# Folded logits copied to SBUF by ScalarE and turned by VectorE later in the loop

## The chip, the cores and the metric

The kernel runs on one core of one Trainium2 chip. A core has TensorE (matmuls, reading SBUF and writing PSUM), VectorE, ScalarE and GpSimd (called POOL in the profile), a queue for DMA transfers (SyncE), the on-chip memory SBUF and the accumulator memory PSUM with its eight banks of 128 x 512 f32. The engines run side by side, each in its own written order, and meet at semaphores: one instruction raises a counter, another engine waits for a value. The metric is the device time of one execution in microseconds (us), the median of several runs.

## The reference

Three blocks in a row: an attention with a decaying state, a gated MLP, and a mixture of experts with 32 slots. The slots' logits are used twice: over all tokens (a softmax down the 3072 tokens) and within a token (a softmax over the 32 slots).

```python
def _attn_ref(r, k, v, w, u):                # 4 x 8 heads, 768 tokens, 48 wide
    for t in range(S):
        cur = np.einsum('bhd,bhe->bhde', u[None] * kt, vt)
        y[:, :, t] = np.einsum('bhd,bhde->bhe', rt, state + cur)
        state = wt[:, :, :, None] * state + np.einsum('bhd,bhe->bhde', kt, vt)

def _moe_ref(x, w_in, w_out):                # 3072 x 384, inner width 2048
    h = x @ w_in
    g = h * np.clip(h + 3.0, 0.0, 6.0) / 6.0
    return g @ w_out

def _moe2_ref(x, phi, w1, w2):               # 8 experts x 4 slots, inner width 1024
    logits = x @ phi
    d = np.exp(logits - logits.max(0, keepdims=True))
    d /= d.sum(0, keepdims=True) + 1e-09
    slot_input = d.T @ x                     # then two matmuls per expert
    c = np.exp(logits - logits.max(1, keepdims=True))
    c /= c.sum(1, keepdims=True) + 1e-09
    return c @ slot_out
```

## The kernel before

**Tiles and stages.** The 768 positions are cut into six chunks of 128 (`C` = 6), each for the four batches (`B` = 4): 24 attention units. Four units make a token group of 512 tokens. The first four units run ahead of the loop. The loop then takes 96 steps (`STEPS`), 16 (`FT`) for each of the six token groups. In step s, with `g, i = divmod(s, FT)`, TensorE computes tile i of the MLP's hidden layer for group g: nine f16 matmuls of 128 x 512 into `hid` (`mlp`, L602; a high and a low half each of weights and x stand in for f32). ScalarE takes the clipped part (`relu_step`, L1473), VectorE multiplies (`gate`, L1075) and turns the product (`turn_gated`, L1096) into a ring of tiles. The matmuls of step s wait for the gate of step s - 2. Beside that, one attention unit of a later group is worked on every four steps (`unit_of`; phases 0 to 3).

**The attention unit on the engines.** Phase 0: TensorE's `score` (L500) waits for the decayed keys and receptances of POOL; VectorE finishes the output of the unit before (`finish_y`, L1035, which waits for POOL's `diag_values`, L1663) and adds its state (L1044). Phase 1: VectorE masks the scores (L1016) and scans a prefix (L962), ScalarE makes their high half (`high_scores`, L1380), and TensorE turns x (`turn_x`, L599), for which it waits for `finish_y`. Phase 2: TensorE turns the keys (L510), ScalarE copies them to SBUF (`copy_keys`, L1394), and TensorE makes the state increment with them (`increment`, L529). Phase 3: TensorE attends (L575 to L592); VectorE scans the suffix (L975), from which POOL decays the keys of the next unit (`decay_keys`, L1678). The loop's increments and key turns end with unit 19, which is worked on in group 3.

**The logits of a group.** `w_out @ phi` is folded into `w_phi`, so the logits come straight from the gated tiles. `add_logits` (L664) adds them up in one PSUM bank, `l_ps`, four tiles at a time, in four parts of 32 rows each. The last four are added in step 0 of the next group. Then, all for group g - 1 and in group g:

- step 1: ScalarE and VectorE split `l_ps` into a high and a low half (L1486, L1104; both lie in the SBUF tile `l_part`, which is a part of `soft3`, "soft" in the profile), and TensorE sums the four parts back into `l_ps` (`fold_logits`, L695, L696), waiting for both halves;
- step 2: VectorE takes the maximum (L1110), ScalarE the exponential (`weigh`, L1497) and from the second group on the factor `alpha` (L1503), and VectorE turns the weights (`turn_weight`, L1141);
- step 2, or step 4 for the last two groups of the five: VectorE turns the logits themselves into SBUF in four 32 x 128 transposes out of `l_ps` (`turn_logits`, L1119), for the second softmax;
- step 3: TensorE gathers the slots (`gather_slots`, L727), 64 matmuls into four banks, one of which is `l_ps` for groups 0 to 2 (for groups 3 and 4 it is `inc_ps`, free by then: `idle_inc`);
- step 4: VectorE adds the slot sums (`add_slots`, L1165);
- step 5: TensorE starts on the next logits in `l_ps`.

So `l_ps` has to be empty for the gather, where that writes it, and for the next logits. TensorE waits for `logits_done` in both places. The sixth group has code of its own.

**What sets the order.** Every engine's order is written out by hand: each engine's block has its own `for s in range(END)` with conditions on the phase, on g and on i. Nothing is rearranged afterwards.

## Time and profile before

| | us |
|---|---|
| median of 3 runs | 411.77 (411.71 to 412.57) |
| profiled execution | 412.07 |
| its span, first to last instruction | 410.1 |
| TensorE busy | 391.4 (95%) |
| VectorE busy | 333.9 (81%) |
| ScalarE busy | 198.4 (48%) |
| POOL busy | 217.5 (53%) |
| mean granted clock of TensorE | 0.992 of full speed |

The loop starts at about 36 us and ends at about 357 us; expert weights and outputs take the rest. A busy share is an average: what an edit is worth is read at the place it touches, from who waits there for whom. A row of the timeline gives the start, the duration, the engine, the line, the operation with output and input, and in square brackets how long the engine had been idle and what released it. On TensorE the durations overlap, since matmuls are pipelined: a 128 x 512 matmul is listed with 0.38 us and the next starts 0.22 later. On ScalarE and VectorE neighbours overlap by up to about 0.1 us too.

### The profile page before, as it was taken

What the parts mean: (1) busy time and instruction counts of PE and PEld (TensorE: products, weight loads), DVE (VectorE), ACT (ScalarE), POOL (GpSimd) and SP (SyncE); (2) the same over time, 40 slices, a digit from 0 to 9 for tenths busy, and PEclk for the clock granted to TensorE, in tenths of its full rate; (3) what the DMA queues carried; (4) which work ended last, traced back from release to release, by engine and by line L of the source; (5) the groups of instructions that cost most, each with busy time, mean ns of one, the idle gap of its engine ahead of it and who ended that gap; (6) DMA issues with size and microseconds to landing.
All of it is one profiled execution on the core that took longest, in us unless ns stands there. A gap on an engine that the chain in (4) does not pass through costs nothing.

```text
span 410.1 us, 10077 instructions
## 1 busy us (share of the span) xinstructions
PE 391.4 (95%) x3977; PEld 210.0 (51%) x3977; DVE 333.9 (81%) x536; ACT 198.4 (48%) x408; POOL 217.5 (53%) x206
## 2 busy tenths in 40 slices
PE   7999999999999999999999999999999999999981
PEld 3885555455455554555554555554444444543430
DVE  7998799998999898998989998989876887661251
ACT  3576355545545757366554556653533234321141
POOL 2444988978468777658774687775650012010000
PEclk9999999999999999999999999999999999999996
DMA  8999412439242134124430331232007199779929
GB/s 236 336 410 315 135 32 97 125 125 363 74 126 76 53 125 128 39 90 126 127 101 28 126 96 58 100 127 59 2 2 305 21 399 408 238 281 417 391 109 356
DMA packets 16542, 69.36 MB, mean 169 GB/s; under 512 B 2160, under 2 KB 3184, under 8 KB 14832
## 3 DMA queue, kind: packets, MB, share of 16 engines
q1 hardware_dynamic: 16496, 68.73, 48.1%
q8 instruction: 31, 0.51, 0.5%
q14 instruction: 15, 0.12, 0.1%
HBM read 64.00 MB, written 4.72 MB: 168 GB/s over the span
## 4 chain that ended last, share of the span: by engine, by line
PE 57%; issue 14%; POOL 12%; DVE 7%; DMA 5%; ACT 2%; SPq 0%; POOLq 0%; DVEq 0%
PE hid L616 10%; PE hid L617 9%; PE hid L618 9%; DMA att<-rkT_dram 4%; PE l_ps L664 4%; PE l_ps L727 3%; PE sc_ps L500 3%; PE hid L886 3%; POOL w_split L1648 2%; POOL att L1690 2%; DVE att L962 2%; POOL att L1634 1%; PE y_ps L599 1%; POOL att L1678 1%; PE inc_ps L529 1%
## 5 line engine op out<-in xcount | busy, mean ns | idle before, releaser
L1473 ACT ACTIVATE relu<-hid,three 128x512 f32<-128x512 f32 x95 | 65.0, 684 | 93.1 <-PE hid L618 92.8
L616 PE MATMUL hid<-x_split,w_split 128*128 128x512 f16 x285 | 108.3, 380 | 0.7 <-DVE gated L1075 0.7
L618 PE MATMUL hid<-x_split,w_split 128*128 128x512 f16 x285 | 108.0, 379 | 0.0
L617 PE MATMUL hid<-x_split,w_split 128*128 128x512 f16 x285 | 108.0, 379 | 0.0
L1075 DVE SCALAR_TENSOR_TENSOR gated<-relu,hid 128x512 f32<-128x512 f32 x95 | 64.7, 681 | 21.4 <-ACT relu L1473 20.5
L1096 DVE STREAM_TRANSPOSE ring<-gated 128x512 f32<-128x512 f32 x96 | 68.3, 711 | 3.3
L1669 POOL TENSOR_TENSOR att<-att 128x1024 f16<-128x1024 f32 x20 | 41.9, 2096 | 30.0 <-ACT att L1380 30.0
L1678 POOL TENSOR_TENSOR att<-att 112x512 f32<-112x512 f32 x21 | 25.5, 1213 | 43.5 <-DVE att L975 33.9
L616 PEld LDWEIGHTS hid<-x_split,w_split 128*128 128x128 f16 x285 | 27.7, 97 | 37.2 <-DVE gated L1075 6.6
L618 PEld LDWEIGHTS hid<-x_split,w_split 128*128 128x128 f16 x285 | 27.8, 98 | 33.7
L617 PEld LDWEIGHTS hid<-x_split,w_split 128*128 128x128 f16 x285 | 27.9, 98 | 24.6
L1429 ACT ACTIVATE x_split<-y_ps 128x384 f16<-128x384 f32 x24 | 11.8, 490 | 40.5 <-PE y_ps L599 40.5
L500 PEld LDWEIGHTS sc_ps<-att 48*128 48x128 f32 x384 | 23.3, 187 | 9.6 <-issue 8.5
L500 PE MATMUL sc_ps<-att 48*128 48x128 f32 x384 | 27.9, 284 | 0.2 <-POOL att L1678 0.2
L727 PE MATMUL sc_ps<-ring,soft 32*32 32x512 f32 x384 | 26.1, 598 | 0.0
L1380 ACT ACTIVATE att<-att 128x1024 f16<-128x1024 f32 x20 | 21.1, 1057 | 9.8 <-DVE att L1016 8.7
L727 PE MATMUL k_ps<-ring,soft 32*32 32x512 f32 x192 | 25.6, 598 | 0.0
L1690 POOL TENSOR_TENSOR att<-att 112x512 f32<-112x512 f32 x19 | 23.5, 1237 | 3.0 <-DVE att L996 3.0
L1016 DVE TENSOR_TENSOR att<-sc_ps,mask 128x1024 f32<-128x1024 f32 x19 | 22.7, 1195 | 0.5 <-issue 0.5
L962 DVE TENSOR_TENSOR_SCAN att<-att 112x517 f32<-112x517 f32 x16 | 22.7, 1419 | 0.0
L1636 POOL TENSOR_TENSOR att<-att 128x384 f32<-128x384 f32 x20 | 20.9, 1045 | 1.6
L664 PE MATMUL l_ps<-gated,w_phi 128*32 128x512 f32 x160 | 21.3, 605 | 0.0
(299 smaller groups left out, 859.2 us busy)
## 6 DMA issues: line engine op xcount, KB each, us to landing
att<-nat_dram SPq DMA_DIRECT2D x20, 576.0 KB, 4.2
att<-rkT_dram SPq DMA_DIRECT2D x22, 448.0 KB, 5.6
att<-wT_dram SPq DMA_DIRECT2D x22, 226.2 KB, 4.7
att<-w_dram SPq DMA_DIRECT2D x3, 1536.0 KB, 9.9
out_dram<-w_split SPq DMA_DIRECT2D x11, 384.0 KB, 3.9
att<-w_dram SPq DMA_DIRECT2D x5, 768.0 KB, 10.4
stage<-w_in_dram SPq DMA_DIRECT2D x2, 1536.0 KB, 14.0
ring<-w_outT_dram SPq DMA_DIRECT2D x1, 3072.0 KB, 15.5
```

What stands on the lines that cost most here:

```text
L500: last = pe.matmul(sc_bank[j][:, cols], k_dec[n % 2][rows, cols], r_dec_of(n)[rows, cols], start=True, stop=True)
L616: pe.matmul(hid[s % 2][:], high, x_high, start=(q == 0), stop=False)
L617: pe.matmul(hid[s % 2][:], high, x_low, start=False, stop=False)
L618: last = pe.matmul(hid[s % 2][:], low, x_high, start=False, stop=(q == KT - 1))
L664: pe.matmul(l_ps[SLOTS * c:SLOTS * (c + 1), :], w_phi[:, i * SLOTS:(i + 1) * SLOTS], gated_tile(g * FT + i), start=(m == 0), stop=(m == 3) ...
L727: ins = pe.matmul(dg_bank_of(g, a)[SLOTS * c:SLOTS * (c + 1), :], weight_T[SLOTS * a:SLOTS * (a + 1), b * SLOTS:(b + 1) * SLOTS], ring_gro ...
L962: nc.vector.tensor_tensor_scan(prefix[0:PD, :], w_rows_of(n)[0:PD, :], mark[0:PD, :], 1.0, ALU.mult, ALU.add).then_inc(prefix_done, 1)
L1075: nc.vector.scalar_tensor_tensor(gated_tile(s), relu_tile(s), 6.0 * GATE, hid[s % 2][:], ALU.min, ALU.mult).then_inc(gated_done, 1)
L1096: nc.vector.transpose(ring_tile(s), gated_tile(s)).then_inc(gated_turned, 1)
L1473: nc.scalar.activation(relu_tile(s), hid[s % 2][:], ACT.Relu, bias=three[:], scale=GATE / H_SCALE)\
L1669: nc.gpsimd.tensor_tensor(scores_lo, scores, scores_hi, ALU.subtract).then_inc(scores_lo_done, 1)
L1690: nc.gpsimd.tensor_tensor(dst, receptance, decay, ALU.mult).then_inc(r_dec_done, 1)
```

## The change

The transposes of the logits read SBUF in place of PSUM and stand elsewhere.

- ScalarE gets `copy_folded`, behind `weigh` in step 2: it copies `l_ps` to `l_part` (128 x 512, f32) and raises `folded_copied`. This is done for groups 0 to 4.
- The gather of groups 0 to 2 and the first `add_logits` of the next group wait for `folded_copied`, no longer for `logits_done`.
- `turn_logits` reads `l_part`. For groups 0, 1 and 2 it moves from step 2 of the next group to step 9, behind the state addition. For group 3 it moves from behind the slot sums in step 4 of group 4 to the last step of group 4, between `gate` and `turn_gated`. For group 4 it stays where it is.
- The next write to `l_part`, in `copy_logit_parts`, waits for `logits_done`.

```diff
@@ add_logits, add_last_logits, gather_slots (TensorE)
-                        pe.wait_ge(logits_done, g)
+                        pe.wait_ge(folded_copied, g)
...
-                    pe.wait_ge(logits_done, C - 1)
+                    pe.wait_ge(folded_copied, C - 1)
...
-                    pe.wait_ge(logits_done, g + 1)
+                    pe.wait_ge(folded_copied, g + 1)
@@ turn_logits (VectorE)
-                dve.wait_ge(weight_done, g + 1)
+                dve.wait_ge(folded_copied, g + 1)
...
-                    tokens = l_ps[rows, :].rearrange("p (t q n) -> p t q n", t=B, q=4)[:, :, a]
+                    tokens = l_part[rows, :].rearrange("p (t q n) -> p t q n", t=B, q=4)[:, :, a]
@@ the loop of VectorE, phase 0
+                    if 1 <= g < C - 2 and i == 9:
+                        turn_logits(g - 1)
@@ phase 1
                         turn_weight(g - 1)
-                        if g - 1 not in idle_inc:
-                            turn_logits(g - 1)
@@ phase 3
                         add_slots(g - 1)
-                        if g == C - 2:
-                            turn_logits(g - 1)
@@ between gate(s) and turn_gated(s)
+                if s == STEPS - FT - 1:
+                    turn_logits(C - 3)
@@ copy_logit_parts, copy_folded, the loop of ScalarE
                     act.wait_ge(folded, g)
+                    act.wait_ge(logits_done, g)
...
+            def copy_folded(g):
+                act.wait_ge(neg_max_done, g + 1)
+                nc.scalar.activation(l_part, l_ps[:], ACT.Copy).then_inc(folded_copied, 1)
...
                         weigh(g - 1)
+                        copy_folded(g - 1)
```

How the instructions stand now, at three places. The line numbers of the changed kernel are one to six higher than those of the one before. `att` is the attention's working memory, `soft` holds `l_part` and the weights, `stats` single columns.

**ScalarE, step 2 of group 2.** Before: the exponential, alpha, the scores' high half, the relu of the step, the copy of the keys.

```order
L1497 ACTIVATE soft<-l_ps,stats 128x512 [waits run_sum_done,neg_max_done]
L1503 ACTIVATE stats<-stats 128x1 [waits acc_added]
L1380 ACTIVATE att<-att 128x1024 [waits y_ready,masked]
L1473 ACTIVATE relu<-hid,three 128x512 [waits hid_ready]
L1394 ACTIVATE att<-k_ps 128x448 [waits inc_ready,k_turned]
```

In the changed kernel, same place:

```order
L1499 ACTIVATE soft<-l_ps,stats 128x512 [waits run_sum_done,neg_max_done]
L1505 ACTIVATE stats<-stats 128x1 [waits acc_added]
L1509 ACTIVATE soft<-l_ps 128x512 [waits neg_max_done]
L1381 ACTIVATE att<-att 128x1024 [waits y_ready,masked]
L1474 ACTIVATE relu<-hid,three 128x512 [waits hid_ready]
L1395 ACTIVATE att<-k_ps 128x448 [waits inc_ready,k_turned]
```

The copy of the logits stands between alpha and the scores' high half.

**VectorE, steps 4 and 5 of group 4.** Before: the slot sums, the transposes, then the gate of step 4, the turn of its tile and the attention output of step 5.

```order
L1165 SCALAR_TENSOR_TENSOR acc<-acc,stats,k_ps 128x512
L1119 STREAM_TRANSPOSE logits<-l_ps 32x128 [waits weight_done]
L1119 STREAM_TRANSPOSE logits<-l_ps 32x128 x3
L1075 SCALAR_TENSOR_TENSOR gated<-relu,hid 128x512 [waits l_ready,relu_done]
L1096 STREAM_TRANSPOSE ring<-gated 128x512 [waits dg_ready,gated_done]
L1035 SCALAR_TENSOR_TENSOR att<-y_ps,att 128x384 [waits x_turned,diag_v_done,y_ready]
```

In the changed kernel the four stand 35 rows later, in step 15 of group 4; the subtraction that ends the piece is that of step 1 of group 5, for which the fold waits:

```order
L1076 SCALAR_TENSOR_TENSOR gated<-relu,hid 128x512 [waits l_ready,relu_done]
L1120 STREAM_TRANSPOSE logits<-soft 32x128 [waits folded_copied]
L1120 STREAM_TRANSPOSE logits<-soft 32x128 x3
L1097 STREAM_TRANSPOSE ring<-gated 128x512 [waits dg_ready,gated_done]
L1076 SCALAR_TENSOR_TENSOR gated<-relu,hid 128x512 [waits l_ready,relu_done]
L1097 STREAM_TRANSPOSE ring<-gated 128x512 [waits dg_ready,gated_done]
L1105 TENSOR_TENSOR soft<-l_ps,soft 128x512 [waits l_hi_done]
```

They moved out of step 4 to a place ahead of two turns and a gate.

**VectorE, steps 9 and 10 of group 3** (groups 1 and 2 alike). Before: attention output, state addition, gate, turn, mask of the scores.

```order
L1035 SCALAR_TENSOR_TENSOR att<-y_ps,att 128x384 [waits x_turned,diag_v_done,y_ready]
L1044 TENSOR_TENSOR att<-att,inc_ps 112x384 [waits state_lo_done,inc_ready]
L1075 SCALAR_TENSOR_TENSOR gated<-relu,hid 128x512 [waits l_ready,relu_done]
L1096 STREAM_TRANSPOSE ring<-gated 128x512 [waits dg_ready,gated_done]
L1016 TENSOR_TENSOR att<-sc_ps,mask 128x1024 [waits scores_lo_done,scores_ready]
```

In the changed kernel:

```order
L1036 SCALAR_TENSOR_TENSOR att<-y_ps,att 128x384 [waits x_turned,diag_v_done,y_ready]
L1045 TENSOR_TENSOR att<-att,inc_ps 112x384 [waits state_lo_done,inc_ready]
L1120 STREAM_TRANSPOSE logits<-soft 32x128 [waits folded_copied]
L1120 STREAM_TRANSPOSE logits<-soft 32x128 x3
L1076 SCALAR_TENSOR_TENSOR gated<-relu,hid 128x512 [waits l_ready,relu_done]
L1097 STREAM_TRANSPOSE ring<-gated 128x512 [waits dg_ready,gated_done]
L1017 TENSOR_TENSOR att<-sc_ps,mask 128x1024 [waits scores_lo_done,scores_ready]
```

The four transposes stand ahead of the step's gate and of the masking.

## Rows read from the trace of the kernel before

**Rows 1.** Stretch of group 1: us; busy PE, PEld, DVE, ACT, POOL; PEclk, DMA, GB/s.

```profile
98.68:154.43 55.75, 55.25 (x610) 30.20 (x607) 50.65 (x82) 31.95 (x66) 39.26 (x38) 1.00 0.34 103
```

**Rows 2.** TensorE's waits over the whole span: us in total, times, longest.

```profile
PE l_ps L727 <- DVE logits L1119: 1.4, 3, 0.5
```

**Rows 3.** Single lines: ns min/median/max, first and last start; last, page part 5.

```profile
L1119 DVE STREAM_TRANSPOSE logits<-l_ps x20: 261/312/324, 106.8 to 325.8; 32x128 f32<-32x128 f32 x20
L1294 DVE STREAM_TRANSPOSE w_phi<-l_ps x1: 687/687/687, 56.9 to 56.9; 128x512 f32<-128x512 f32 x1
L1141 DVE STREAM_TRANSPOSE soft<-soft x5: 683/698/712, 106.2 to 320.7; 128x512 f32<-128x512 f32 x5
L962 DVE TENSOR_TENSOR_SCAN att<-att x16: 1215/1326/2737, 76.5 to 287.8; 112x517 f32<-112x517 f32 x16
L1473 ACT ACTIVATE relu<-hid,three 128x512 f32<-128x512 f32 x95 | 65.0, 684 | 93.1 <-PE hid L618 92.8
```

**Rows 4.** Timeline by engine, steps 2 and 3: first row group 1, others group 3.

```profile
104.99 1.06 ACT L1380 ACTIVATE att<-att 128x1024 f16<-128x1024 f32 x1 [0.49 <-DVE att L1016]
...
215.40 0.69 ACT L1497 ACTIVATE soft<-l_ps,stats 128x512 f32<-128x512 f32 x1 [0.55 <-DVE stats L1099]
215.99 0.28 ACT L1503 ACTIVATE stats<-stats 128x1 f32<-128x1 f32 x1
216.53 1.06 ACT L1380 ACTIVATE att<-att 128x1024 f16<-128x1024 f32 x1 [0.26 <-DVE att L1016]
...
218.07 0.54 ACT L1394 ACTIVATE att<-k_ps 128x448 f32<-128x448 f32 x1
...
218.39 1.25 DVE L1119 STREAM_TRANSPOSE logits<-l_ps 32x128 f32<-32x128 f32 x4
...
218.66 0.67 PE L529 MATMUL inc_ps<-att 128*64 128x48 f32 x16
219.79 0.63 PE L727 MATMUL l_ps<-ring,soft 32*32 32x512 f32 x4 [0.47 <-DVE logits L1119]
```

**Rows 5.** Timeline of group 4, steps 4 to 9, VectorE and then TensorE.

```profile
282.26 1.28 DVE L1119 STREAM_TRANSPOSE logits<-l_ps 32x128 f32<-32x128 f32 x4
...
289.60 0.69 DVE L1075 SCALAR_TENSOR_TENSOR gated<-relu,hid 128x512 f32<-128x512 f32 x1 [0.35 <-ACT relu L1473]
...
285.51 0.55 PE L599 MATMUL y_ps<-ident,att 128*128 128x128 f32 x3 [0.44 <-DVE att L1035]
...
290.35 0.39 PE L616 MATMUL hid<-x_split,w_split 128*128 128x512 f16 x1 [0.41 <-DVE gated L1075]
...
295.71 1.16 PE L500 MATMUL sc_ps<-att 48*128 48x128 f32 x16 [0.18 <-POOL att L1678]
```

**Rows 6.** Timeline of group 3 from step 10, by engine, to TensorE's first of group 4.

```profile
247.03 0.54 ACT L1394 ACTIVATE att<-k_ps 128x448 f32<-128x448 f32 x1
...
248.67 0.67 PE L529 MATMUL inc_ps<-att 128*64 128x48 f32 x16
...
247.17 0.69 DVE L1075 SCALAR_TENSOR_TENSOR gated<-relu,hid 128x512 f32<-128x512 f32 x1 [0.28 <-ACT relu L1473]
...
252.13 1.18 POOL L1678 TENSOR_TENSOR att<-att 112x512 f32<-112x512 f32 x1 [1.70 <-DVE att L975]
...
254.38 1.16 PE L500 MATMUL sc_ps<-att 48*128 48x128 f32 x16
...
259.71 0.69 DVE L1075 SCALAR_TENSOR_TENSOR gated<-relu,hid 128x512 f32<-128x512 f32 x1
...
260.74 0.38 PE L616 MATMUL hid<-x_split,w_split 128*128 128x512 f16 x1
```

**Rows 7.** Timeline at the start of group 5: gate, low half of the logits, fold.

```profile
315.29 0.69 DVE L1075 SCALAR_TENSOR_TENSOR gated<-relu,hid 128x512 f32<-128x512 f32 x1 [0.51 <-ACT relu L1473]
...
316.65 0.65 DVE L1104 TENSOR_TENSOR soft<-l_ps,soft 128x512 f16<-128x512 f32 x1
...
317.45 0.38 PE L695 MATMUL l_ps<-soft,fold 128*128 128x512 f16 x1
```

More of the change, by code:

```diff
@@ L310, in build_program @@
         nat_logits_ready = sem("nat_logits_ready")
+        folded_copied = sem("folded_copied")
         logits_done = sem("logits_done")
```

## The prediction

> **What bounds the kernel now.** The table of stretches, cut at the second step of a group, comes first: loop group 1 takes 55.75 us, TensorE is busy for 55.25 of them and VectorE for 50.65, and the granted clock is 1.00, the upper level of 2.4 GHz [rows 1]. So an edit on another engine pays only where TensorE waits for that engine. The list of waits comes second; of the copy of the logits it names one wait of TensorE, 1.4 us in 3 waits, at most 0.5 each [rows 2]. They are the starts of the slot gathers in step 3 of groups 1, 2 and 3. Third, the timeline around each place from which the four transposes go, and each to which they come; there I compare the moment at which TensorE wants a result with the moment at which it is there.
>
> A step's matmuls need the gated product of two steps before. "Step i of group g" is the loop's own count, from 0. All instructions of an engine run in their written order, so an insertion delays everything behind it until that engine next waits for something.
>
> **Part 1: the gather no longer waits for the transposes (groups 1 to 3).** The four transposes take 1.25 us from 218.39 to 219.64, and the gather starts at 219.79 after an idle 0.47 [rows 4]. After the change it wants the ScalarE copy instead. The exponential starts at 215.40 and alpha's 0.59 behind it, though it lasts 0.69 in the rows: neighbours overlap by 0.1. Alpha lasts 0.28, so the copy starts at 215.99 + 0.18 = 216.17; the copy has the shape of the relu, the mean of which is 684 ns [rows 3], so the next instruction may start at 216.17 + 0.58 = 216.75. The copy is ready at 216.85, 2.5 us before the gather. But the instruction behind it, the high half of the scores, ran at 216.53 [rows 4], and is pushed by 0.22 us. So are the relu and the copy of the keys (218.07) behind it, and TensorE's state increment (218.66) starts as soon as those keys are there. The gather therefore wins 0.47 - 0.22 = 0.25 us in groups 2 and 3. In group 1 there is no alpha, and the copy fits into the 0.49 us in which ScalarE waits for the masked scores [rows 4] and what the exponential leaves before, so all of its 0.46 is won. Sum **0.96 us**; bounds 0.7 (pushed in all three) and 1.4 (no push) [rows 2]. VectorE also runs step 2 earlier by 1.28 us, but its gates were not late there, and TensorE gets nothing more from it.
>
> **Part 2: group 4, step 4.** Here the transposes (1.28 us from 282.26) stand behind the slot sums in a stretch where VectorE is late, and three waits of TensorE follow within 14 us: 0.44 for the finished attention output of step 5, 0.41 for the gate of step 6, 0.18 for the decayed keys, which POOL makes behind a scan of VectorE [rows 5]. Without the transposes VectorE is 1.28 us earlier, more than the three together, so they go: 1.03 us. The refill of an emptied matmul queue is not in the three numbers, and VectorE has 0.25 us more to give; I take 0.07 of it. What is late next: the gate of step 6, now 289.60 to 290.29, would be ready at 289.0 [rows 5] against a TensorE that wants it at 290.35 - 1.03 = 289.3, and then VectorE's scan again, within 0.1 us. **1.1 us**; bounds 0.6 (only one of the larger waits goes) and 1.28 (all the removed work).
>
> **Part 3: the transposes in step 9 of groups 1, 2 and 3.** VectorE is given 4 transposes. From PSUM one lasts 312 ns, median; the 128x512 transpose took 687 ns from PSUM and 698 from SBUF [rows 3]. I take equal cost, 1.28 us, as the block in group 4 lasted [rows 5]. All behind them move by it: the gate, the masking, so ScalarE's high scores and relu, so the copy of the keys. At that place of group 3 the keys are copied by 247.57 and TensorE wants them at 248.67: 1.10 us to spare. The relu was already 0.28 behind VectorE (its gate waited), so about 1.0 to 1.1 of the 1.28 arrives: hidden, with nothing left over. POOL's decayed keys are done at 253.31 and wanted at 254.38: 1.07 to spare, the same verdict [rows 6]. The delay then goes around from VectorE's scan through POOL to the next attention output and is not lost by step 14. There the gate starts at 259.71 and is done at 260.40, and TensorE wants it at 260.74, 0.34 later. With 1.0 arriving this is a stall of 0.66 us; VectorE enters step 9 somewhat earlier than now, since it lost 1.28 us in step 2 and TensorE only won 0.25; most of that is eaten by waits for relus, and I take 0.25 of it as left. So 0.4 us lost in group 3. In groups 1 and 2 TensorE has the turn of the keys and the increment in step 15 as well, before it wants that gate; the increment's 0.67 us [rows 4] alone are more than the 0.66 missing, and the delay is hidden. **-0.4 us**; bounds 0 and -1.3 (0.66, and 0.2 in each of three groups should the transposes take longer).
>
> **Part 4: the transposes in step 15 of group 4.** The next gate waited 0.51 us for its relu [rows 7]; that much of the 1.28 is hidden, and a few hundredths are won since the turn of the gated tile no longer waits for its gate. The subtraction that makes the low half of the logits moves from 316.65 by some 0.6, to end at 317.9 instead of 317.30, and TensorE starts the fold at 317.45; 0.1 us of that gap is slack at most. **-0.5 us**; bounds 0 and -0.8 (only the relu's 0.51 is hidden). Group 4's own logits are still turned in group 5, step 4: no change. The copy in group 5 pushes a relu by 0.6 us whose gate is not wanted until the gather's end 4 us later.
>
> One weighing by itself. The Trainium skill, "VectorE: DVE Perf Modes", section on the TRN2 errata, gives a Vector instruction 58 cycles of fixed cost from SBUF and 120 from PSUM at 0.96 GHz. By it, an estimate, each transpose would be 65 ns shorter from SBUF, the four 0.26 us. The pair of 687 and 698 ns [rows 3] speaks against it. It would make of the sum what the second case below makes of it.
>
> **Sum.** 0.96 + 1.10 - 0.40 - 0.50 = 1.16 us. The profiled execution took 412.07 us, 410.1 of span and 1.97 around it, and would become 410.9; it is 0.30 above the median of 411.77, which becomes **410.6 us**. Behind the loop all of the chain goes on from TensorE, and the weight loads are released by TensorE's progress, so nothing there gives the gain back.
>
> **The ways it could go.**
> 1. As summed, 410.6 us (410.1 to 411.3 by itself). Chance 0.45, of which 0.10 lie within 0.2% of before.
> 2. Short transposes. Some of the twenty took 261 ns [rows 3]; were all as short from SBUF, four are 1.04 instead of 1.25 us, and with the spread of VectorE's lateness both stalls shrink by about 0.25: gain 1.65, **410.1 us**. Against it stands the equal pair of long transposes. Chance 0.15. The skill's page named above would say the same.
> 3. The gain is taken back. The waits in group 4 are replaced by waits for relus or for POOL, or the push on ScalarE eats the gathers' gain: parts 1 and 2 give half, 1.03, against the same 0.9 of loss: **411.6 us**. For it: both stretches have VectorE and POOL within 0.1 us of TensorE afterwards. This is also the case in which moving the transposes does not free what it says. Chance 0.28.
> 4. Slower: the transposes now read SBUF while POOL and ScalarE do. The one scan of VectorE with two SBUF inputs that meets POOL spreads from 1215 ns over a median of 1326 to 2737 [rows 3]. If the block grows to x us, TensorE loses 3 (x - 1.1) in step 11 or 13 of three groups and x - 0.7 at the fold, against gains of 2.06: zero at x = 1.5, and slower by 0.2% from x = 1.7, 0.43 us a transpose. At x = 1.75 it is **412.7 us**. Against it: the five long transposes from SBUF are steady, 683 to 712 ns [rows 3]. Chance 0.12.
>
> **How the numbers follow.** What a measurement of this kernel can tell from no change is about 0.2%, 0.8 us. Faster by more: 0.35 + 0.15 = 0.50. Within it: 0.10 + 0.26 = 0.36. Slower: 0.12 + 0.02 = 0.14. The bounds of the four parts, not all bad or good at once, reach from a gain of 2.1 to a loss of 0.4: the range is 409.7 to 412.2 us. It leaves out the slow case and the best ends.
>
> **What would show it.** Right: the gathers' row names no logits any more; the state increment of groups 2 and 3 starts 0.2 us later behind the masking; no wait of TensorE for the attention output in group 4; a wait of about 0.4 us for a gate at the start of group 4 and of about 0.5 at the fold of group 5; the transposes at 0.31 us each; groups 1 to 3 each 0.3 to 0.5 us shorter. Wrong: transposes over 0.4 us, waits of TensorE for keys in step 11 or for POOL in step 13 of groups 1 to 3, or group 4 not about 1 us shorter.

## The result

| | before | changed |
|---|---|---|
| median, same chip | 411.75 (411.47 to 412.57) | 410.04 (409.88 to 411.12) |
| profiled execution | 412.07 | 410.12 |
| its span | 410.1 | 408.4 |
| TensorE / VectorE / ScalarE / POOL busy | 391.4 / 333.9 / 198.4 / 217.5 | 391.8 / 330.9 / 199.8 / 217.5 |

The ratio is 0.9963, 95% interval 0.9949 to 0.9978: faster by 1.5 us, or by 1.7 by the medians. A second comparison, among the runs below, gave 410.36 against 411.60, ratio 0.9961 (0.9931 to 0.9991).

**The profile after.** TensorE's waits over the whole span, in us: total, times, longest.

```profile
PE hid L617 <- DVE gated L1076: 0.7, 2, 0.4
PE y_ps L600 <- DVE att L1036: 0.6, 1, 0.6
...
PE l_ps L696 <- DVE soft L1105: 0.4, 1, 0.4
PE inc_ps L530 <- ACT att L1395: 0.4, 2, 0.2
```

The same view of the kernel before had, beside the row of [rows 2]:

```profile
PE y_ps L599 <- DVE att L1035: 1.0, 2, 0.6
...
PE hid L616 <- DVE gated L1075: 0.7, 2, 0.4
```

The gather's wait for the logits is gone. The attention output is waited for once less, the gate as long as before but elsewhere. The wait of 0.2 for POOL's decayed keys is gone too. New are the last two: the fold of group 5 waits for the low half, and the increments in step 3 of groups 2 and 3 wait for the keys. Two short waits in the first 8 us (L651, 0.4 and 0.3 in the kernel before) come and go between executions of one kernel: the repeat a2_change_again has one of them, the first profile of the changed kernel none. They have nothing to do with the change.

The transposes and the copy as groups (ns min/median/max, first and last start):

```profile
L1120 DVE STREAM_TRANSPOSE logits<-soft x20: 257/303/307, 130.3 to 324.0; 32x128 f32<-32x128 f32 x20
...
L1509 ACT ACTIVATE soft<-l_ps x5: 584/587/588, 104.2 to 318.4; 128x512 f32<-128x512 f32 x5
```

Against 312 ns in [rows 3] a transpose from SBUF is 9 ns shorter, and not 65 as in the estimate that the prediction weighed. The copy takes 0.59 us.

Timeline of the changed kernel, steps 2 and 3 of group 3, which answers [rows 4]: ScalarE, then TensorE.

```profile
214.26 0.69 ACT L1499 ACTIVATE soft<-l_ps,stats 128x512 f32<-128x512 f32 x1 [0.55 <-DVE stats L1100]
214.85 0.28 ACT L1505 ACTIVATE stats<-stats 128x1 f32<-128x1 f32 x1
215.03 0.59 ACT L1509 ACTIVATE soft<-l_ps 128x512 f32<-128x512 f32 x1
215.51 1.06 ACT L1381 ACTIVATE att<-att 128x1024 f16<-128x1024 f32 x1
...
217.63 0.67 PE L530 MATMUL inc_ps<-att 128*64 128x48 f32 x16 [0.17 <-ACT att L1395]
218.23 0.63 PE L728 MATMUL l_ps<-ring,soft 32*32 32x512 f32 x4
```

Between the exponential and the high half of the scores there were 216.53 - 215.40 = 1.13 us before and are 1.25 now: the push is 0.12. The gather starts with no wait of its own.

Timeline from step 9 of group 3 to the start of group 4, which answers [rows 6]: VectorE, TensorE at its increment, at its score and at the first matmul of group 4.

```profile
241.03 1.25 DVE L1120 STREAM_TRANSPOSE logits<-soft 32x128 f32<-32x128 f32 x4
...
258.97 0.68 DVE L1076 SCALAR_TENSOR_TENSOR gated<-relu,hid 128x512 f32<-128x512 f32 x1
...
247.12 0.67 PE L530 MATMUL inc_ps<-att 128*64 128x48 f32 x16
...
252.83 1.16 PE L501 MATMUL sc_ps<-att 48*128 48x128 f32 x16
...
259.79 0.38 PE L617 MATMUL hid<-x_split,w_split 128*128 128x512 f16 x1 [0.44 <-DVE gated L1076]
```

Increment and score do not wait; the hidden tile does, 0.44 us for the gate.

Timeline of group 4 and of the start of group 5, which answers [rows 5, 7]: TensorE's turn of x in step 6, which takes up the attention output of step 5; the gate and the transposes in step 15; the low half; the fold.

```profile
284.05 0.55 PE L600 MATMUL y_ps<-ident,att 128*128 128x128 f32 x3
...
311.07 0.69 DVE L1076 SCALAR_TENSOR_TENSOR gated<-relu,hid 128x512 f32<-128x512 f32 x1 [0.51 <-ACT relu L1474]
311.68 1.25 DVE L1120 STREAM_TRANSPOSE logits<-soft 32x128 f32<-32x128 f32 x4
...
314.91 0.65 DVE L1105 TENSOR_TENSOR soft<-l_ps,soft 128x512 f16<-128x512 f32 x1
...
315.71 0.38 PE L696 MATMUL l_ps<-soft,fold 128*128 128x512 f16 x1 [0.41 <-DVE soft L1105]
```

The wait of 0.44 for the attention output is gone, as are those of step 8 (0.41, for the gate of step 6) and of step 9 (0.18, for the decayed keys), and the fold of group 5 waits 0.41.

**The ledger.** Every group has two marks on TensorE: the first matmul of the fold (L695, in the changed kernel L696) and the first of the gather (L727, L728). Where two kernels have the same order between two marks, the distance comes out the same to 0.02 us, while the first fold of all starts anywhere from 99.9 to 103.7 us. So all that follows is counted from the first fold to the last gather:

| kernel | fold to gather, groups 1, 2, 3, 4 | gather to fold, groups 1, 2, 3, 4 | first fold to last gather |
|---|---|---|---|
| before | 7.61 7.62 7.63 6.57 | 48.15 48.15 47.06 44.03 | 221.23 |
| changed | 7.08 7.21 7.21 6.56 | 48.15 48.16 47.67 43.25 | 219.70 |
| e1_copy_old_places | 7.07 7.22 7.21 6.57 | 48.16 48.15 47.07 42.96 | 218.82 |
| e2_g4_moved_only | 7.08 7.21 7.22 6.57 | 48.16 48.15 47.06 43.24 | 219.10 |
| e3_step14 | 7.08 7.20 7.20 6.57 | 48.16 48.16 47.68 42.70 | 219.16 |
| e4_halves_in_idle | 7.07 7.20 7.20 6.57 | 48.16 48.16 47.07 43.24 | 219.08 |
| e6_copy_early | 7.09 7.09 7.09 6.60 | 48.15 48.16 47.67 43.24 | 219.50 |
| e7_copy_twice | 7.60 7.84 7.84 6.57 | 48.16 48.15 47.67 43.24 | 221.48 |
| e8_both_idle | 7.08 7.20 7.20 6.56 | 48.16 48.15 47.08 42.71 | 218.55 |
| b1_later_pool | 7.59 7.63 7.62 6.57 | 48.16 48.15 47.06 44.04 | 221.23 |
| c1_meeting_made | 7.07 7.20 7.21 6.56 | 48.16 48.16 47.07 44.11 | 219.95 |
| e9_all_three | 7.08 7.09 7.09 6.57 | 48.16 48.15 47.07 42.71 | 218.33 |

(The last column also has 4.41 us from the fold of group 5 to its gather, in all kernels alike.) The change is worth 1.53 us in it; the span's 1.7 has 0.21 more, since the first fold came 0.21 earlier (100.42 against 100.63), less some hundredths behind the last gather. Nothing was changed ahead of the first fold.

### The profile page after: what moved, and what is told of

It reads as the page before. It is cut to its first block, busy times and chain, and to the rows that moved or that the text cites. A ratio compares the mean times of both kernels' runs of the same rounds, so it can differ in the third digit from the quotient of the medians.

```text
span 408.4 us, 10082 instructions
## 1 busy us (share of the span) xinstructions
PE 391.8 (96%) x3977; PEld 210.4 (52%) x3977; DVE 330.9 (81%) x536; ACT 199.8 (49%) x413; POOL 217.5 (53%) x206
## 4 chain that ended last, share of the span: by engine, by line
PE 29%; POOL 29%; issue 27%; DMA 5%; DVE 4%; ACT 1%; SPq 1%; POOLq 0%; DVEq 0%
DMA att<-rkT_dram 5%; PE hid L617 4%; POOL att L1697 4%; PE hid L619 4%; PE hid L618 4%; POOL att L1641 4%; POOL att L1643 4%; POOL att L1670 3%; POOL att L1701 3%; POOL spare L1705 3%; PE hid L887 3%; POOL att L1662 3%; POOL w_split L1655 2%; PE inc_ps L728 1%; POOL att L1685 1%
## 5 line engine op out<-in xcount | busy, mean ns | idle before, releaser
L728 PE MATMUL sc_ps<-ring,soft 32*32 32x512 f32 x384 | 26.1, 598 | 0.0
L728 PE MATMUL k_ps<-ring,soft 32*32 32x512 f32 x192 | 25.7, 598 | 0.0
```

Of the source, the lines that this page charges most:

```text
L728: ins = pe.matmul(dg_bank_of(g, a)[SLOTS * c:SLOTS * (c + 1), :], weight_T[SLOTS * a:SLOTS * (a + 1), b * SLOTS:(b + 1) * SLOTS], ring_gro ...
```

## The experiments

**The copy alone: e1_copy_old_places.** The changed kernel with the transposes back in step 2 and in step 4 of group 4, still out of SBUF.

```diff
-                    if 1 <= g < C - 2 and i == 9:
-                        turn_logits(g - 1)
...
                         turn_weight(g - 1)
+                        if g - 1 not in idle_inc:
+                            turn_logits(g - 1)
...
                         add_slots(g - 1)
+                        if g == C - 2:
+                            turn_logits(g - 1)
...
-                if s == STEPS - FT - 1:
-                    turn_logits(C - 3)
```

> The change with all its ScalarE copies and with the waits on them, but the four transposes of each group stand where they stood before (step 2 in groups 1 to 3, step 4 in group 4); they read SBUF. Theory (the gain is four separate terms): only the gathers' gain is left, 0.5 us in group 1 and 0.4 in groups 2 and 3, so 1.35 us under before, 410.4 us, and 0.35 over the change; the three waits in group 4 (0.4, 0.4, 0.2) are back, and neither the wait for the gate at the start of group 4 nor that at the fold of group 5 is there. Rival (the gathers' gain needs VectorE freed in step 2, since the gate, the sum and the slot sums behind the transposes then come too late): the gain appears at the gather and is lost again by the next fold, 411.3 us or more.

Measured: 409.77 us against 411.89, ratio 0.9943 (0.9931 to 0.9955). In the table it beats the change by 0.88 us (218.82 against 219.70); the intervals of the two ratios overlap. Part 1 is all there (7.07, 7.22, 7.21), part 3 is gone (47.07), and group 4, where nothing on VectorE was moved, went from 44.03 to 42.96. That was in no theory: of its three waits only the 0.18 for the decayed keys was back.

**What happened in group 4.** VectorE and POOL in step 3 of group 4, in the kernel before:

```profile
275.08 1.26 DVE L1152 SCALAR_TENSOR_TENSOR stats<-stats 128x1 f32<-128x1 f32 x1
...
275.14 1.19 POOL L1690 TENSOR_TENSOR att<-att 112x512 f32<-112x512 f32 x1
```

The same place in e1_copy_old_places:

```profile
273.40 0.23 DVE L1153 SCALAR_TENSOR_TENSOR stats<-stats 128x1 f32<-128x1 f32 x1
...
273.57 1.19 POOL L1697 TENSOR_TENSOR att<-att 112x512 f32<-112x512 f32 x1
```

A product of single columns, both inputs in SBUF, took 1.26 us and ended at 276.34, with POOL's operation (276.33) that had begun 0.06 us behind it. Where POOL begins 0.17 behind, it takes 0.23. Below, a product that stands for POOL's operation in this way is called the meeting. The copy pushes the scores' high half on ScalarE by 0.12 us, POOL's products come behind that, and so the product gets through ahead of them. The Trainium skill, "SBUF — State Buffer", section "SBUF: two separate sides", says that a VectorE operation with two SBUF inputs and a GpSimd operation that reads SBUF take a port pair exclusively for the whole instruction and that the loser fully blocks; the two ends at the same moment agree. By its rule the one that starts first wins; in these records the loser is listed 0.06 us ahead.

**Group 4 alone: e2_g4_moved_only.** Groups 1 to 3 as in the run above, the block of group 4 in step 15 as in the change.

> The change, with the transposes of groups 0 to 2 back in step 2 of the next group (reading SBUF), and those of group 3 in step 15 of group 4 as in the change. Theory (the move to step 9 buys nothing and costs 0.6 us at the start of group 4): 0.6 us under the change, 409.4 us. Rival (step 9 is where VectorE has time, and its lateness behind the slot sums in steps 4 to 8 is what the move takes away): not faster than the change, 410.0 us or more.

Measured: 409.89 us, ratio 0.9948 (0.9936 to 0.9960). Group 4 has 43.24 where e1 has 42.96: from where it stood, with the copy made, the move to step 15 loses 0.28 us. The move to step 9 costs what the theory said: without it the table has 219.10, 0.60 less than the change.

**One step earlier: e3_step14.** The change with the block of group 4 ahead of the gate of step 14.

```diff
+                if s == STEPS - FT - 2:
+                    turn_logits(C - 3)
                 if 1 < s < STEPS - 1:
                     gate(s)
-                if s == STEPS - FT - 1:
-                    turn_logits(C - 3)
```

> The change, with the transposes of group 3 one step earlier, in step 14 of group 4 ahead of the gate, where VectorE waits 1.54 us for a relu. Theory: the 0.41 us at the fold of group 5 go and nothing takes their place, 409.6 us. Rival (the fold is held by ScalarE's high half or by TensorE's own order, within 0.2 us): 409.9 us.

Measured: 409.79 us, ratio 0.9967 (0.9940 to 0.9994; its runs reach up to 415.46), and 42.70 in group 4, 0.55 less than in the change, so the fold's wait goes as the theory said. In step 14 the block lies in VectorE's idle time ahead of three gates, of which each waits for its relu:

```profile
308.38 1.23 DVE L1120 STREAM_TRANSPOSE logits<-soft 32x128 f32<-32x128 f32 x4
310.00 0.69 DVE L1076 SCALAR_TENSOR_TENSOR gated<-relu,hid 128x512 f32<-128x512 f32 x1 [0.39 <-ACT relu L1474]
...
311.94 0.69 DVE L1076 SCALAR_TENSOR_TENSOR gated<-relu,hid 128x512 f32<-128x512 f32 x1 [0.51 <-ACT relu L1474]
```

**Two halves in steps 9 and 13: e4_halves_in_idle.** Two transposes each, ahead of the attention output, for which VectorE waits for POOL. `turn_logits_half` is `turn_logits` for two of the four transposes.

```diff
+                    if 1 <= g < C - 2 and i in (9, 13):
+                        turn_logits_half(g - 1, (i - 9) // 4)
                     if is_unit(n - 1):
                         finish_y(n - 1)
...
-                    if 1 <= g < C - 2 and i == 9:
-                        turn_logits(g - 1)
```

> The change, with the four transposes of groups 0 to 2 split: two ahead of the attention output of step 9 and two ahead of that of step 13, where VectorE waits 0.6 us for POOL each time. Theory (what reaches the start of group 4 is the block less the idle time ahead of it): all hidden, the wait of 0.44 us for the gate at the start of group 4 is gone, 0.6 us under the change, 409.4 us. Rival (the loop of VectorE, ScalarE and POOL has no idle time of its own, and what VectorE waits for moves with it): at most half of it, 409.8 us.

Measured: 409.60 us, ratio 0.9949 (0.9930 to 0.9968); group 3 is back at 47.07, so all of part 3's loss is avoided, as in the theory.

**The step 9 block twice: e5_step9_doubled.** `turn_logits` of groups 1 to 3 writes its four transposes a second time, behind a wait for the first four.

> The change, with the four transposes of step 9 done twice in each of groups 1 to 3 (the second time behind a wait for the first), 2.5 to 2.7 us in place of 1.25. Theory (the room is 1.1 us of slack between the copied keys and the state increment): TensorE waits for the keys in step 11 of all three groups, 1.1 to 1.4 us each, and the later gate is no later against TensorE than in the change: 3.3 to 4 us over the change, 413.3 to 414. Rival (the delay is soaked up by idle time of VectorE as the single block was in groups 1 and 2): under 1.5 us in all, 411.5 at most.

Measured: 414.04, 414.46 and 415.30 us at a granted clock of 0.99, ratio 1.0057 (1.0040 to 1.0073); the fourth execution, the profiled one, took 421.05 at 0.942. So the profile's distances aren't comparable with those of the table; its waits name the place (TensorE):

```profile
PE inc_ps L531 <- ACT att L1402: 2.2, 3, 0.7
```

Three waits of 0.7 for the keys, one a group: one block of 1.25 us raises no wait for the keys in step 11, a second one does. At the lower clock TensorE wants the keys later, so 0.7 is not their length at the full clock; there the median is 4.1 us above the change's 410.36 in the second comparison, or 1.4 a group, a little over what the theory gave. The rival, under 1.5 us in all, is out.

**The copy ahead of the exponential: e6_copy_early.** The copy waits for the fold, and the maximum on VectorE for the copy.

```diff
             def group_maximum(g):
-                dve.wait_ge(folded, g + 1)
+                dve.wait_ge(folded_copied, g + 1)
...
             def copy_folded(g):
-                act.wait_ge(neg_max_done, g + 1)
+                act.wait_ge(folded, g + 1)
...
+                    if 1 <= g < C and i == 2:
+                        copy_folded(g - 1)
                     if is_unit(n - 1):
                         high_x(n - 1)
                     if 1 <= g < C and i == 2:
                         weigh(g - 1)
-                        copy_folded(g - 1)
```

> The change, with ScalarE's copy ahead of the exponential, at the head of step 2, where ScalarE waits 1.28 us for the turned x; VectorE's maximum waits for the copy, since both read one bank. Theory (in groups 2 and 3 the copy behind alpha pushes the scores' high half and with it the keys and the gather by 0.1 us each): the gather of groups 2 and 3 gains 0.1 us more each, 409.8 us. Rival (the maximum now waits, and with it the exponential and the weights): the turned weights come last, no gain or a loss of up to 0.3 us a group, 410.0 to 411.

Measured: 410.35 us, ratio 0.9957 (0.9944 to 0.9969). The pushes are gone: 7.09 in all three groups, 0.12 less in groups 2 and 3. The table has 0.20 less than for the change, as in the theory, but the medians show no gain. And POOL, no longer pushed, again starts 0.06 us behind VectorE's product. VectorE and POOL in group 2 and in group 3:

```profile
163.86 1.26 DVE L1153 SCALAR_TENSOR_TENSOR stats<-stats 128x1 f32<-128x1 f32 x1
...
163.92 1.19 POOL L1698 TENSOR_TENSOR att<-att 112x512 f32<-112x512 f32 x1
...
219.11 0.22 DVE L1153 SCALAR_TENSOR_TENSOR stats<-stats 128x1 f32<-128x1 f32 x1
...
219.17 1.22 POOL L1698 TENSOR_TENSOR att<-att 112x512 f32<-112x512 f32 x1
```

At the same distance the product lost once and got through once. And where it lost, group 2 still has 48.16: the delay is hidden there.

**The copy twice: e7_copy_twice.** A second copy behind a wait for the first.

> The change, with ScalarE's copy done twice in each of five groups, the second behind a wait for the first, 0.6 to 0.7 us more in step 2. Theory (what ScalarE does in step 2 pushes the scores' high half, the relu, the keys, the increment and so the gather one for one, once the 0.5 us of waiting for the masked scores are used up): 0.6 us later gathers in groups 1 to 3, 1.8 us over the change, 411.8 us; groups 4 and 5 lose nothing. Rival (a quarter of ScalarE's time is idle there and takes it): under 0.5 us in all.

Measured: 412.24 us, the median of nine (a tenth took 418.29), ratio 1.0012 (0.9999 to 1.0026). The gathers go to 7.60, 7.84, 7.84: 0.52 us more in group 1 and 0.63 in groups 2 and 3, for 0.62 us more on ScalarE (216.31 to 216.93 between the two copies). Where alpha has used up ScalarE's idle time, the push counts in full: TensorE waits for the keys. In all it is 1.78 us (221.48 against 219.70), the theory's 1.8.

```profile
PE inc_ps L531 <- ACT att L1396: 2.2, 3, 0.8
```

**Both idle places: e8_both_idle.** e3_step14 and e4_halves_in_idle together.

> The change with both better places: halves ahead of the attention outputs of steps 9 and 13 for groups 0 to 2, and step 14 of group 4 for group 3. Theory: the two gains add, 0.6 + 0.4 us, 409.0 us. Rival (they overlap in what TensorE then waits for): 409.4 us.

Measured: 409.09 us against 411.98, ratio 0.9930 (0.9916 to 0.9943): the lowest median of all, with 47.08 and 42.71. The two gains add (0.60 and 0.55; 219.70 to 218.55).

**Is it the meeting or the moved work?** In group 4 the change took away two delays of VectorE at once, the meeting (its successor starts 1.18 us behind it instead of 0.15: 1.03) and the transposes (1.28). Three kernels separate them. The first is the kernel before with POOL's chain later, b1_later_pool:

```diff
                     nc.scalar.activation(alpha, run_neg[1 - g % 2], ACT.Exp, bias=run_neg[g % 2], scale=-1.0).then_inc(alpha_done, 1)
+                if g == C - 3:
+                    for spare_column in (6, 60, 62):
+                        nc.scalar.activation(stats[:, spare_column:spare_column + 1], three[:], ACT.Copy)
```

> The kernel before, with transposes where they were and no copy, and one thing added: behind the weight's alpha in step 2 of group 4 ScalarE writes three 128x1 columns that nobody needs yet, some 0.18 us each by the distance of 214.85 and 215.03 in the changed kernel. ScalarE was idle for 0.26 us there (the exponential at 271.22 in the kernel before), so that exponential, and with it GpSimd's products of step 3, come about 0.2 to 0.3 us later. Nothing is taken off VectorE. The theory of the meeting (VectorE's 128x1 product of the sums at 275.08 stood for 1.26 us because GpSimd's 112x512 operation began 0.06 us behind it): the product takes 0.22 to 0.23 us again, gather to fold of group 4 shrinks from 44.03 to 43.0 to 43.2, all else stays, and the time is 410.7 to 410.9 us against 411.75. The rival (what group 4 gained in the changed kernel came from the four transposes taken out of step 4): the product still takes 1.26 us or its end is hidden, gather to fold stays 44.0 to 44.1, and the time is 411.7 to 411.9 us.

Measured: 411.72 us, the median of eleven (a twelfth took 418.06), ratio 0.9992 (0.9966 to 1.0018). It decides nothing. ScalarE at the added columns, then VectorE and POOL at the meeting:

```profile
270.73 0.38 ACT L1506 ACTIVATE stats<-three 128x1 f32<-128x1 f32 x3
271.09 1.06 ACT L1380 ACTIVATE att<-att 128x1024 f16<-128x1024 f32 x1
...
274.95 1.26 DVE L1152 SCALAR_TENSOR_TENSOR stats<-stats 128x1 f32<-128x1 f32 x1
...
275.00 1.19 POOL L1693 TENSOR_TENSOR att<-att 112x512 f32<-112x512 f32 x1
```

The three columns took 0.36 us (270.73 to 271.09) and not 0.54, which just filled the gap: from the exponential to the scores' high half it is 1.13 us, as before. So POOL was not pushed, and the meeting stands.

The second makes the meeting in the kernel that had lost it, c1_meeting_made: e1_copy_old_places with a small sum ahead of the weight's sum in group 4.

```diff
                     if g >= 1 and i == 3:
+                        if g == C - 2:
+                            nc.vector.tensor_reduce(stats[:, 6:7], weight[:, 0:P], AX_X, ALU.add)
                         sum_weight(g - 1)
```

> The other way round: the kernel with the copy on ScalarE and the transposes in their old places (409.77 us, gather to fold of group 4 42.96), and one 128x128 sum more on VectorE ahead of the sum of the weight in step 3 of group 4, some 0.25 us, so that the 128x1 product comes to start behind GpSimd's 112x512 operation and not 0.17 us ahead of it. The theory of the meeting: the product starts at or behind GpSimd's operation and ends with it, some 1.2 us in all or a wait of as much before it, gather to fold of group 4 grows by 0.9 to 1.2 to 43.9 to 44.1, and the time is 410.7 to 411.0 us. The rival (a VectorE that is 0.25 us later there costs 0.25 us): the product takes 0.22 us, gather to fold is 42.96 to 43.2, and the time is 409.8 to 410.0 us.

Measured: median 410.97 us, 1.2 above e1_copy_old_places on another chip; against the kernel before, whose runs spread from 410.01 to 415.91 there, the ratio is 0.9993 (0.9958 to 1.0028). The distance says it sharper: group 4 grows from 42.96 to 44.11, as the theory of the meeting had it; the rival allowed 43.2. VectorE and POOL:

```profile
276.15 0.24 DVE L1264 TENSOR_REDUCE stats<-soft 128x1 f32<-128x128 f32 x1
276.31 0.67 DVE L1150 TENSOR_REDUCE stats<-soft 128x1 f32<-128x512 f32 x1
277.02 1.19 DVE L1153 SCALAR_TENSOR_TENSOR stats<-stats 128x1 f32<-128x1 f32 x1
...
277.00 1.19 POOL L1699 TENSOR_TENSOR att<-att 112x512 f32<-112x512 f32 x1
```

The added sum holds VectorE for 0.16 us; the product, now 0.02 behind POOL, stands until POOL ends. So 0.16 us of added work cost 1.15.

The third keeps the meeting and has the transposes elsewhere, e9_all_three: e8_both_idle with the copy early, as in e6_copy_early.

> Both transposes in idle places (409.09 us) and the copy ahead of the exponential, behind the fold's last matmul, with the group maximum behind the copy. Each of the three gave its part alone: the fold to gather times 7.09 instead of 7.20 in groups 2 and 3, 0.22 us in all, so 408.8 to 408.9 us. The rival, from the run with the copy early alone: GpSimd is no longer pushed, the 128x1 product and GpSimd's 112x512 operation begin 0.06 us apart again, and in any group where GpSimd comes out ahead the product takes 1.26 us, which would give 409.7 to 410.0 us.

Measured: median 409.26 us, ratio 0.9952 (0.9921 to 0.9983), no faster than e8_both_idle's 409.09 as far as the medians tell, though it has 0.22 us less from the first fold to the last gather. In groups 3 and 4 the product lost again, here in group 4:

```profile
273.79 1.26 DVE L1163 SCALAR_TENSOR_TENSOR stats<-stats 128x1 f32<-128x1 f32 x1
...
273.85 1.18 POOL L1708 TENSOR_TENSOR att<-att 112x512 f32<-112x512 f32 x1
```

and yet group 4 takes 42.71. The expectation that a lost meeting costs 1 us was wrong: alone it costs nothing. The four cases of group 4 fit one number, about 1.0 us that VectorE can be late in steps 3 and 4 before TensorE loses anything:

| kernel | delay of VectorE | gather to fold | above 42.71 | delay less 1.0 |
|---|---|---|---|---|
| e9_all_three: meeting | 1.03 | 42.71 | 0.00 | 0.03 |
| e1_copy_old_places: transposes | 1.25 | 42.96 | 0.25 | 0.25 |
| before: both | 2.31 | 44.03 | 1.32 | 1.31 |
| c1_meeting_made: both and a sum | 2.37 | 44.11 | 1.40 | 1.37 |

(c1: 0.16, 0.96 by the distance from 277.02 to 278.13 less 0.15, and 1.25.)

The same subtraction, made at each place where TensorE waits, says who sets the 1.0. Counted from the gather by the first hidden-layer matmul behind each wait, the kernel before is 0.50 us behind e8_both_idle after the turn of x in step 6, 1.07 at step 8 and 1.33 behind the score of step 9; c1 is 0.58, 1.15 and 1.40 behind; e1 is level until step 9 and then 0.25 behind. So VectorE can be late by 1.8 us for the attention output, by 1.2 for the gate of step 6, and by 1.0 for POOL's decayed keys, which step 9 takes up: the tightest of the three sets what is lost in the end, and it is not the one that TensorE is seen to wait for first.

**The change once more: a2_change_again.**

> The change as it is, once more beside the others: 410.0 us, VectorE's 128x1 product of the sums at about 274.1 takes 0.23 us in group 4, fold to gather 7.08, 7.20, 7.20, 6.57, gather to fold 48.16, 48.16, 47.67, 43.24. If the product's length is a matter of chance even at 0.17 us apart, it is 1.2 us here in some group, and the time about 411 us.

Measured: 410.36 us. Its distances are those of the changed kernel within 0.02 us, and the product takes 0.23 us in all three groups in which POOL's operation is near.

## Why the prediction was right

The forecast was a gain of 1.16 us, to 410.6; it was 1.53 in the ledger and 1.7 by the medians, to 410.04. The likeliest case came true, at its better edge. Term by term:

- **Part 1**, forecast 0.96: **1.36** (0.53, 0.41, 0.42). The mechanism held. Two sizes were off. The price of the copy was taken from the relu's 684 ns, and it took 587, so the push was 0.12 and not 0.22: 0.20 us in two groups. And the gather's wait is worth more than its listed 0.46 or 0.47: from the increment to the gather it was 1.13 us in all three groups before (218.66 to 219.79 in group 3) and is 0.60 now (217.63 to 218.23), 0.53 less. That is 0.06 a group, or 0.18 us; and 0.53 - 0.12 is the 0.41 measured.
- **Part 2**, forecast 1.1: **1.32** (44.03 to 42.71, the kernels with the block in an idle place). The step held: the three waits go when 1.28 us of transposes go, and e9_all_three shows it with the meeting still there. Mis-sized is what comes on top of the listed waits, taken as 0.07: the waits of 0.44, 0.41 and 0.18 cost 0.50, 0.57 and 0.25 by the starts of the matmuls behind them, 0.29 more than listed. What the step did not see is why VectorE was late: 1.03 of it was one instruction on single columns that stood for a POOL operation. That row was in the trace. The change dissolves it as well, by its push on ScalarE, and then the transposes in step 4 cost only 0.25. So the gain has two causes of which either would have brought most of it, and e1_copy_old_places collects 1.07 of the 1.32 without moving anything.
- **Part 3**, forecast -0.4: **-0.61**, all in group 3, as said; groups 1 and 2 hide it (48.15 and 48.16). The place was right, the first gate of group 4, and the delay that arrives there too: the gate stood 19.91 us behind the first matmul of step 9 (239.80 to 259.71) and stands 20.72 behind it (238.25 to 258.97), 0.81 later where the forecast had 1.0 less 0.25. Mis-sized is the slack of 0.34: TensorE's first matmul starts 0.14 us behind the end of the gate (259.65 to 259.79), which leaves 0.20, and 0.81 - 0.20 is what was lost. The listed 0.44 is short of it because the wait is counted from the listed end of the matmul before (258.97 + 0.38), whose successor would have started after 0.22. Of the keys and of the score nothing was lost, as said; the keys are copied 0.17 us ahead of the increment of step 11 now, where they had 1.10 to spare.
- **Part 4**, forecast -0.5: **-0.54** (43.25 against 42.71). The fold waits 0.41 for the low half.

Short transposes (case 2) did not come: 303 ns against 312. Nor did the growth of case 4: 257 to 307, although POOL is at work beside the block of step 9 without a break of over 0.1 us (240.78 to 243.91; the block is at 241.03 to 242.28). The scan's long executions, which case 4 leant on, come from POOL, as the last section shows; the transposes beside POOL did not share that. Of the signs named, the gathers' row, the missing wait in group 4, the wait at the first gate and the fold's came as written. The increment's came at half its size: it starts 0.10 us later behind the masking (215.28 to 218.66 before, 214.15 to 217.63 now) and not 0.2, and TensorE waits 0.17 for the keys.

The sum of errors, 0.4 + 0.22 - 0.21 - 0.04, was 0.37 us on the good side. That it is no more is luck in part: the gains were 0.62 too low and the losses 0.25 too low, and most of both has one root, that a wait was priced by its listed length and a slack by the end of the instruction. The larger miss is about what the change is made of: once the copy is there, the moves as they were made cost 0.29 us in group 4 and 0.60 in group 3 (219.70 against 218.82); moved to idle places they are worth 0.27 (218.55).

## What to carry to other kernels

Before a stall is credited to the block ahead of it, look for instructions far above the usual length of their kind: one of 1.26 us instead of 0.22 was half of the lateness here, and went with a shift of 0.1 us on a third engine. Work taken off a late engine is worth its length less what the engine has to spare, so of two delays in one stretch the second may be worth almost nothing once the first is gone. Price a wait by the starts of the matmuls on both sides of it, before and without it, not by its listed length: here 1.03 us of listed waits cost 1.32. A block that has to go somewhere belongs ahead of an instruction that waits for another engine anyway, split if the idle piece is short: that was worth 1.15 us here (e8_both_idle against the change, 219.70 to 218.55), as much as the change was expected to bring.

## What the runs showed of the hardware

- VectorE's 128x1 product of two SBUF columns beside a POOL operation of 1.19 us: with POOL 0.05 or 0.06 us behind it, it took 1.25 or 1.26 us in five of eight meetings (before, b1_later_pool, e6_copy_early once in three, e9_all_three twice in three) and 0.22 in the other three, so that near it is left to chance or to less than the records resolve; in those three POOL's operation is listed with 1.22. With POOL 0.17 to 0.21 behind, the product took 0.23 to 0.27 in all twenty-three; with POOL 0.02 ahead, 1.19.
- The prefix scan, two SBUF inputs as well, has the same cause in plain sight. In the kernel before it runs sixteen times. Eight begin with POOL idle and take 1.22 us. Eight begin inside a POOL operation, and each ends 1.09 or 1.10 us behind the end of that operation, as such scans do in all fourteen profiles: it takes 1.43 or 1.44 where POOL has 0.34 left, 1.52 or 1.53 where it has 0.43 or 0.44, and 2.74 where it has 1.65, the longest execution in [rows 3]. POOL's next operation, which takes 2.00 us by itself, begins before that scan ends and takes 2.93:

```profile
76.52 2.74 DVE L962 TENSOR_TENSOR_SCAN att<-att 112x517 f32<-112x517 f32 x1
...
76.52 1.65 POOL L1648 TENSOR_TENSOR w_split<-stage,w_split 128x768 f16<-128x768 f32 x1
78.11 2.93 POOL L1669 TENSOR_TENSOR att<-att 128x1024 f16<-128x1024 f32 x1
```

- ScalarE's copy of 128 x 512 f32 from PSUM to SBUF takes 587 ns where the relu with a bias column of the same shape takes 684.
- What stays open: in the last comparison the kernel before spreads more than the others. 14 of its 35 executions there have spans of 408.3 to 409.1 us, about 1 us under the usual 410.0, and so have 3 of the 12 of b1_later_pool; of its 15 executions in the comparison before that, one has. A product that gets through in some executions would give 1.07 us less and fits, but no profile shows it: both profiles of kernels with that order (before and b1_later_pool) had it lose. If it is so, the change is worth 1.5 us against the one form and, as an estimate from the table (221.23 - 1.07 against 219.70), 0.5 against the other.
